# Transfers moved between queues, filler matmuls moved, and one routing stage shifted by a unit in a fused attention and mixture-of-experts kernel

## The reference

```python
# attention: q, k, v of (4, 8, 576, 64)
scores = scale * q @ k.T
scores = np.where(scores >= max(scores) - tau, scores, -1e9)
attn = softmax(scores)                 # over the keys
x = (attn @ v)                         # -> 2304 tokens x 512
# mixture of 8 experts, one expert for each token
logits = (x / |x|) @ (emb / |emb|).T / tau
e = argmax(logits); gate = softmax(logits)[e]
y = gate * (relu(x @ w1[e]) @ w2[e])   # 512 -> 1024 -> 512
# dense block
h = y @ w_in                           # 512 -> 2048
out = (max(h, 0) + alpha * min(h, 0)) @ w_out
```

## Time and profile before

| | us |
|---|---|
| time, median of 3 runs | 1015.94 |
| the three runs | 1015.75, 1015.94, 1016.86 |
| time of the profiled execution | 1015.94 |
| its span (first to last instruction) | 1014.3 |
| PE busy | 1002.7 |
| DVE busy | 528.1 |
| ACT busy | 390.8 |
| POOL busy | 337.4 |

### The profile page before, as it was taken

How to read it: one execution, slowest core, us unless ns; L and a number is a source line. 1 busy time by engine, 2 the same in 40 slices (tenths; PEclk the granted TensorE clock), 3 DMA queues, 4 the chain that set the end, 5 groups by cost and what they waited for, 6 DMA issues and landing times.

```text
span 1014.3 us, 19467 instructions
## 1 busy us (share of the span) xinstructions
PE 1002.7 (99%) x6541; PEld 882.8 (87%) x6542; DVE 528.1 (52%) x1206; ACT 390.8 (39%) x814; POOL 337.4 (33%) x446
## 2 busy tenths in 40 slices
PE   8999999999999999999999999999999999999997
PEld 7988998998988788888888889999899999998996
DVE  6888888888987422222212237544444444444442
ACT  5777777777767232222223223321121211111111
POOL 3333334222131789999954542010010100100101
PEclk9999999999999999999999999999999999999999
DMA  5866776776662555665563335000000000000000
GB/s 133 225 153 167 185 190 172 185 187 174 148 178 52 217 196 203 210 210 192 188 201 128 129 130 155 6 32 32 1 32 32 32 12 19 31 0 0 32 1 31
DMA packets 103744, 116.69 MB, mean 115 GB/s; under 512 B 70380, under 2 KB 70412, under 8 KB 103156
## 3 DMA queue, kind: packets, MB, share of 16 engines
q1 hardware_dynamic: 88404, 87.52, 31.5%
q10 hardware_dynamic: 11120, 13.97, 4.3%
q0 software_dynamic: 4144, 14.20, 3.9%
HBM read 68.53 MB, written 19.12 MB: 86 GB/s over the span
## 4 chain that ended last, share of the span: by engine, by line
PE 95%; POOL 2%; DVE 2%; issue 1%; DMA 0%; ACT 0%; POOLq 0%; SPq 0%; DVEq 0%; ACTq 0%
PE bank L790 82%; PE bank L793 13%; POOL ring L690 1%; DVE neg_max L1563 0%; POOL ring L688 0%; DMA qraw<-in_q 0%; DVE probs L1571 0%; POOLq L89 0%; DVE q_st L1588 0%; POOL x_sorted L731 0%; POOL out L783 0%; DVE k_both L1592 0%; ACT probs L1302 0%; DVE k_st L1592 0%; ACT o_row L1527 0%
## 5 line engine op out<-in xcount | busy, mean ns | idle before, releaser
L790 PE MATMUL bank<-x_hi,ring 128*128 128x384 f32 x768 | 210.5, 337 | 0.0
L790 PE MATMUL bank<-ring,g_hi 128*128 128x512 f32 x576 | 179.1, 392 | 0.0
L1504 ACT ACTIVATE g_hi<-act 128x384 fp32r<-128x384 f32 x96 | 50.4, 525 | 298.9 <-DVE act L1947 296.5
L690 POOL TENSOR_TENSOR ring<-stage,ring 128x2048 fp32r<-128x2048 f32 x32 | 147.2, 4600 | 4.8 <-POOL ring L688 0.2
L790 PEld LDWEIGHTS bank<-x_hi,ring 128*128 128x128 f32 x768 | 140.2, 188 | 3.5
L1944 DVE TENSOR_SCALAR neg<-bank,alpha_col 128x384 f32<-128x384 f32 x96 | 59.2, 617 | 150.8 <-PE bank L790 150.8
L790 PE MATMUL bank<-x_lo,ring 128*128 128x384 f32 x384 | 128.9, 336 | 0.0
L1563 DVE TENSOR_REDUCE neg_max<-bank 128x1 f32<-128x576 f32 x144 | 104.5, 753 | 40.9 <-PE bank L790 39.8
L1302 ACT ACTIVATE probs<-bank,neg_max 128x576 f32<-128x576 f32 x144 | 103.3, 741 | 51.5 <-DVE neg_max L1563 51.4
L790 PEld LDWEIGHTS bank<-ring,g_hi 128*128 128x128 f32 x576 | 106.8, 188 | 18.7 <-DVE g_lo L1895 0.3
L790 PE MATMUL bank<-k_st,q_st 128*128 128x288 f32 (+5 forms) x696 | 114.7, 306 | 0.8 <-DVE probs L1571 0.6
(11 more groups left out here) (204 smaller groups left out, 1406.2 us busy)
## 6 DMA issues: line engine op xcount, KB each, us to landing
stage<-in_moe_w SPq DMA_DIRECT2D x26, 1024.0 KB, 5.3
k_st<-k_both SPq DMA_DIRECT2D x60, 288.0 KB, 4.8
x_row<-x_sorted ACTq DMA_DIRECT2D x23, 296.0 KB, 3.2
stage<-in_moe_w SPq DMA_DIRECT2D x12, 512.0 KB, 5.8
y_sorted<-y_row ACTq DMA_DIRECT2D x21, 256.5 KB, 2.9
q_st<-q_hi SPq DMA_DIRECT2D x30, 160.0 KB, 2.8
q_st<-q_lo SPq DMA_DIRECT2D x30, 160.0 KB, 2.9
qraw<-in_q SPq DMA_DIRECT2D x16, 256.0 KB, 3.1
```

Source lines behind the costliest of these rows:

```text
L690: nc.gpsimd.tensor_tensor(lo, src, hi.bitcast(F32), ALU.subtract).then_inc(piece_lo, 2)
L790: return nc.tensor.matmul(dst, lhsT, rhs, start=start, stop=stop)
L1504: nc.scalar.activation(g_hi[f % 3][:, :], act2[f % 2][:, :], ACT.Copy).then_inc(g_hi_ready, 1)
```

## The change

The changes are these.

- **Start.** The 4 filler matmuls on `vraw` and their semaphore are gone. POOL clears both `vraw` after `qraw` and `kraw`.
- **Unit 0 of pair 0.** The last part of the preparation of pair 1 stood before `turn_last_keys` with 4 fillers behind it. It now stands at the end of the unit, and the 4 fillers are gone.
- **The load of the opening slot** (`x_row`) is issued by SP behind the four loads of `vraw` of pair 15, and no longer by ACT in unit 2 of pair 14.
- **Routing group 2.** Its steps on DVE, its rank on PE and its scatters on POOL each stand one unit later. Two small operations of DVE (`open_gap`, `iota_pos`) move from unit 4 of pair 14 to the end of group 2's steps.
- **After attention.** The zeros of expert 1 and the loads of slots 0 and 1 move from ACT to SP. PE transposes slot 0 (`turn_slot(0)`) behind the whole opening slot, with one filler matmul ahead of it and three behind it.

```diff
+WARM, WARM_SPLIT = 1, 3
...
-STEP_AT = ((0, 1, 2, 3, 4, 5, 6, 8, 8, 9),) * 2 + ((-1, -1, 0, 0, 1, 1, 2, 4, 4, 5),)
-RANK_UNIT = (4, 4, 0)
-SCATTER_AT = ((10, 11, 12, 13),) * 2 + ((6, 6, 7, 7, 8),)
+STEP_AT = ((0, 1, 2, 3, 4, 5, 6, 8, 8, 9),) * 2 + ((0, 0, 1, 1, 2, 2, 3, 5, 5, 6),)
+RANK_UNIT = (4, 4, 1)
+SCATTER_AT = ((10, 11, 12, 13),) * 2 + ((7, 7, 8, 8, 9),)
...
 @block.sync
                     load_v(n + 1, 1 - par)
+                    if n == PAIRS - 2:
+                        sp.wait_ge(scattered_open, 16 * OPEN_TILES)
+                        sp.dma_start(x_row[:, :], x_sorted[0:P, :]).then_inc(open_in, 16)
...
-            for e in (0, *range(2, EXPERTS)):
+            for e in range(EXPERTS):
                 if e == 2:
+                    sp.wait_ge(rows_ready, 1)
+                    rows = [sp.value_load(slot_row[0:1, i:i + 1], ...) for i in range(2)]
+                    for z in range(2):
+                        sp.wait_ge(zeroed[z], 16)
+                    sp.wait_ge(open_turned, 1)
+                    sp.wait_ge(open_squared, 1)
+                    sp.wait_ge(scattered, 16 * (TT - OPEN_TILES))
+                    sp.dma_start(x_row[:, :], x_sorted[ds(rows[0], P), :]).then_inc(xs_in, 16)
+                    sp.wait_ge(table_ready, 1)
+                    sp.dma_start(x_row1[:, :], x_sorted[ds(rows[1], P), :]).then_inc(xs1_in, 16)
                     sp.wait_ge(xs_in, 16)
...
 @block.gpsimd
-            nc.gpsimd.memset(vraw[1][:, MAIN:MAIN + 2, :, :], 0.0).then_inc(fill_ready, 1)
             for t in (*qraw, *kraw):
                 nc.gpsimd.memset(t[:, MAIN, :, :], 0.0)
-            nc.gpsimd.memset(vraw[0][:, MAIN:MAIN + 2, :, :], 0.0).then_inc(const_ready, 1)
+            for t in vraw:
+                last = nc.gpsimd.memset(t[:, MAIN:MAIN + 2, :, :], 0.0)
+            last.then_inc(const_ready, 1)
...
 @block.tensor
-            pe.wait_ge(fill_ready, 1)
-            blank = vraw[1][:, MAIN, :, :].rearrange("p h d -> p (h d)")
-            for _ in range(FILL // 2):
-                mm(bank[:, T_BANK[0], 0:P], blank, blank, True, True)
             pe.wait_ge(const_ready, 3)
...
                     turn_probs(n, j, 0)
-                    if (n, j) == (0, 0):
-                        pe.wait_ge(split_lo, GROUPS_PREP + len(SECOND_BANKS))
-                        prep(1, 1, 0, 2)
-                        busy(FILL // 2, M_BANK)
                     turn_last_keys(n, j)
...
-                    if job and (n, j) != (0, 0):
+                    if job:
...
             open_second(range(0, 4), True)
-            turn_slot(0)
             pe.wait_ge(open_hT_lo, 2)
             open_second(range(4, FC), True, stop=True).then_inc(slots_done, 1)
+            def warm_up(n):
+                for _ in range(n):
+                    mm(bank[:, M_BANK, :], ring[:, 0, 0:P], ring[:, 0, 0:D], True, True)
+            warm_up(WARM)
...
 slot_first(i)
+                if static(i):
+                    turn_slot(0)
+                    warm_up(WARM_SPLIT)
                 pe.wait_ge(piece_lo, e * PIECES + DC)
...
 @block.scalar
-                    if (n, j) == (PAIRS - 2, 2):
-                        act.wait_ge(scattered_open, 16 * OPEN_TILES)
-                        act.dma_start(x_row[:, :], x_sorted[0:P, :]).then_inc(open_in, 16)
...
-                if s == 0:
-                    act.wait_ge(route_const, 9)
-                    act.wait_ge(zero_ready, 1)
-                    row = act.value_load(zero_at[0:1, 1:2], ...)
-                    act.dma_start(x_sorted[ds(row, P), :], zero_row[:, :]).then_inc(zeroed[1], 16)
-                else:
-                    act.wait_ge(rows_ready, 1)
-                    row = act.value_load(slot_row[0:1, 0:1], ...)
...
-            for e in range(2):
-                act.wait_ge(zeroed[e], 16)
-            act.wait_ge(open_squared, 1)
-            act.wait_ge(scattered, 16 * (TT - OPEN_TILES))
-            act.dma_start(x_row[:, :], x_sorted[ds(row, P), :]).then_inc(xs_in, 16)
-            act.wait_ge(table_ready, 1)
-            load_slot(1)
```

More of the change, by code:

```diff
@@ L241, in build @@
         const_ready = sem("const_ready")
-        fill_ready = sem("fill_ready")
         taus_in = sem("taus_in")
@@ L617, in _ @@
             sp.wait_ge(zero_ready, 1)
-            for e in (0, *range(2, EXPERTS)):
+            for e in range(EXPERTS):
                 if e == 2:
+                    sp.wait_ge(rows_ready, 1)
+                    rows = [sp.value_load(slot_row[0:1, i:i + 1], min_val=0, max_val=EXPERTS * CAP + P) for i in range(2)]
+                    for z in range(2):
[6 more added lines that the diff above has]
+                    sp.dma_start(x_row1[:, :], x_sorted[ds(rows[1], P), :]).then_inc(xs1_in, 16)
                     sp.wait_ge(xs_in, 16)
@@ L1046, in open_second @@
                 return last
-            H_BANK, HT_BANK, X_BANK, Y_BANK = (0, 1), (2, 3), 4, 5
-            def turn_slot(i):
-                wait_row(pe, i)
-                if not static(i):
-                    pe.wait_ge(xs_lo, i)
-                row = row_of(i)
-                for c in range(DC):
-                    last = turn(bank[:, X_BANK, c * P:(c + 1) * P], row[:, c * TURNED + EXPERTS:c * TURNED + EXPERTS + P])
-                last.then_inc(xs_turned, 1)
             def turn_params():
@@ L1099, in _, with turn_slot @@
             open_second(range(0, 4), True)
-            turn_slot(0)
             pe.wait_ge(open_hT_lo, 2)
             open_second(range(4, FC), True, stop=True).then_inc(slots_done, 1)
+            def warm_up(n):
+                for _ in range(n):
+                    mm(bank[:, M_BANK, :], ring[:, 0, 0:P], ring[:, 0, 0:D], True, True)
+            warm_up(WARM)
+            H_BANK, HT_BANK, X_BANK, Y_BANK = (0, 1), (2, 3), 4, 5
+            def turn_slot(i):
+                wait_row(pe, i)
+                if not static(i):
+                    pe.wait_ge(xs_lo, i)
+                row = row_of(i)
+                for c in range(DC):
+                    last = turn(bank[:, X_BANK, c * P:(c + 1) * P], row[:, c * TURNED + EXPERTS:c * TURNED + EXPERTS + P])
+                last.then_inc(xs_turned, 1)
             flat = ring[:, :, :].rearrange("p r n -> p (r n)")
@@ L1397, in _ @@
                 nc.scalar.activation(h_row[:, s * D:(s + 1) * D], bank[:, OPEN_H[s], :], ACT.Relu).then_inc(open_relu, 1)
-                if s == 0:
-                    act.wait_ge(route_const, 9)
-                    act.wait_ge(zero_ready, 1)
-                    row = act.value_load(zero_at[0:1, 1:2], min_val=0, max_val=EXPERTS * CAP)
-                    act.dma_start(x_sorted[ds(row, P), :], zero_row[:, :]).then_inc(zeroed[1], 16)
-                else:
-                    act.wait_ge(rows_ready, 1)
-                    row = act.value_load(slot_row[0:1, 0:1], min_val=0, max_val=EXPERTS * CAP + P)
                 act.wait_ge(open_hT, s + 1)
@@ L1686, in route_step @@
                     V.tensor_copy(hot_of(g + 1)[:, 1:EXPERTS, 0], cum_of(g)[:, 1:EXPERTS, nt])
-                    then(V.scalar_tensor_tensor(out=hot_of(g + 1)[:, 0:1, 0], in0=r_open[:, :], scalar=0.0, in1=cum_of(g)[:, 0:1, nt],
-                                                op0=ALU.max, op1=ALU.add))
+                    V.scalar_tensor_tensor(out=hot_of(g + 1)[:, 0:1, 0], in0=r_open[:, :], scalar=0.0, in1=cum_of(g)[:, 0:1, nt],
+                                           op0=ALU.max, op1=ALU.add)
+                    then(V.tensor_scalar(open_gap[:, :], r_open[0:1, :], 0.0, -float(P), ALU.max, ALU.mult))
+                    dve.wait_ge(route, count[0])
+                    then(V.tensor_scalar(iota_pos[:, :], iota_i[:, :], float(P), open_gap[0:1, 0:1], ALU.mult, ALU.add))
             def pair(n, par, half):
@@ L1725, in pair @@
                         constants()
-                    if (n, j) == (PAIRS - 2, UNITS - 1):
-                        dve.wait_ge(route, count[0])
-                        then(V.tensor_scalar(open_gap[:, :], r_open[0:1, :], 0.0, -float(P), ALU.max, ALU.mult))
-                        dve.wait_ge(route, count[0])
-                        then(V.tensor_scalar(iota_pos[:, :], iota_i[:, :], float(P), open_gap[0:1, 0:1], ALU.mult, ALU.add))
                     for g in range(3):
```

## The result

The changed kernel takes 1023.62 us (median of 4 runs, 1022.81 to 1024.05), the kernel before 1016.40 us in the runs beside it (1015.75 to 1016.91). The ratio is 1.0069, 95% interval 1.0055 to 1.0085: 7.2 us slower, where 3.1 us were predicted. The profiled execution of the changed kernel took 1024.61 us; its span is 1022.9 us, 8.6 us more than that of before.

The account below looks back on a forecast made before the run. PE, busy 99% of the span, was taken as the bound. Terms 2.5 (opening slot's load) + 0.6 (start) + 0 + 0 + 0 = +3.1 us on 1015.94 gave 1019.0 us, range 1016.4 to 1021.4.

Parts of the forecast that it names:

- unit 0: Unit 0 of pair 0: removed fillers and moved transposes lie ahead of PE's wait for DVE's probs; 0 us.
- The clock falls: Rival: PE standing about 3 us for x_row may return to 1.2 GHz; price 2 us, 1021.0 us; chance 0.12.
- The load of the opening slot: Pair 14, main term: SP issues x_row later, it lands at 310.4, PE stands 2.6 us; +2.5 us net.
- the scatter's 1.3 us: Pair 14: one more group 2 scatter in the full DMA stretch, 1.3 us more, backlog ending near 310.3.
- The start: Kernel start: later first matmul delays the clock's rise past the q transposes; +0.6 us, bounds 0 and +1.1.
- Group 2: Routing group 2 one unit later: same instructions, DVE has room; 0 us, bounds -0.3 and +0.3.
- After attention: Passage to the slots: slot 0 ends within or close to PE's 0.52 us wait for POOL; 0, bounds 0 and +0.9.
- a sign: Passage to the slots: PE's start of slot 1 would still wait for POOL.
- early landing rival: Pair 14: SP through at 305.6 to 306, rows by 308.8, PE stands 0.5 to 1 us; 1017.2 or 1016.4; chance 0.20.

Follow-up runs that it names:

- b_late_first: Kernel before with routing group 2 one unit later and the opening slot's load by SP ahead of the four vraw loads; 1018.03 us, ratio 1.0015.
- b_load: Kernel before with only the opening slot's load moved to SP, behind the four vraw loads of pair 15; 1018.55 us, ratio 1.0016.
- b_open: Kernel before with the opening slot's load by SP behind the vraw loads and routing group 2 one unit later; 1021.52 us, ratio 1.0051.
- b_unit0: Kernel before with pair 1's last preparation part at the end of unit 0 of pair 0, its 4 fillers gone; 1016.98 us, ratio 1.0016.

## Why the prediction fell short

The forecast was 4.1 us short: 7.2 us were measured and 3.1 predicted. About 1.6 us of this are the clock in unit 0, about 1.6 the clock at the stand, and 0.9 the stand itself (3.4 instead of 2.5).

- **The clock is the step that failed.** "PE idles some 1 us there instead; I expect no fall of the clock from it" was wrong: unit 0 costs 1.6 us alone (0.2 to 3.0), not 0. And the rival *The clock falls* was given 0.12 although its price of 2 us was near the 1.3 to 1.6 measured. The argument against it, that the clock never fell in this trace with a longest stand of 0.73 us, was no evidence about a stand of 3 us, which before never had while there was work. And the same trace has a longer stand, at its end, which the prediction did not look at:

```profile
1007.34 0.39 PE L790 MATMUL bank<-ring,g_lo 128*128 128x512 f32 x1
```

```profile
1012.00:1013.00 1.00, 0.00 (x0) 0.00 (x0) 0.00 (x0) 0.00 (x0) 0.00 (x0) 0.56 0.00 0
```

The first row is PE's last matmul, the second the stretch in which the clock falls, at 1012.1 (from 1011 to 1012 it is still 1.00). That is 4.4 us after the matmul's end (in `b_late_first` 2.1 us after it). So that a stand of some microseconds can bring the clock down could be seen before anything was run. All five profiled executions with a bare stand of 3.3 to 3.7 us for `x_row` show a half clock that begins in the stand or within 0.9 us behind it; the two with 2.3 and 1.4 us do not. Stand and clock should have been one term of 4 to 5 us. As the clock does not fall in every execution, it would still have been a chance and not a certainty.
- **The load of the opening slot** was predicted at +2.5, from a landing at 310.4. The mechanism was right: PE stands for `x_row`, released by the DMA. Its size was too small. The sum held SP's issue at 307.09 and put the scatter's 1.3 us on the landing. The runs show it the other way: SP's issues ahead of the load take 1.1 us longer, and the landing keeps its 3.1 to 3.3 us. `b_load` does land at 310.4 (issue at 307.11, transposes at 310.45, stand 2.26), but without the scatter that the prediction had counted in, so this agreement is luck; with group 2 the stand is 3.4.
- The Trainium skill, "TensorE: Matmul & The Clock Gate", Part 1, says that the slow clock is the default and is returned to when PE idles. The prediction used that page for the start and not for the stand. The stands of 3.4 us agree with it. The same Part 1 tells of a kernel whose short idle times between groups of matmuls made its clock swing; the front of this kernel, with 0.69 and 0.96 us of idle, is nearer to that.
- **The start**: predicted +0.6, measured 0.9 (0.0 to 1.8), and 0.6 as the average of the traces. The size was right, and the reason in the main: with a late first matmul six of seven traces have slow q transposes, with an early one two of ten.
- **Group 2** was priced at 0 ± 0.3 for DVE's steps. No run has it alone; in `b_late_first` 1.5 us were lost and 1.37 of them are the stand, which leaves nothing to speak of for the steps. Its scatters are worth 1.1 us of stand.
- **After attention**: predicted 0, measured 0.7 (-0.2 to 1.6) in and nothing out. Not told from 0. PE no longer waits for POOL at slot 1 in the changed kernel, which the prediction had named as a sign.
- The parts sum to 2.6 + 5.1 + 0.7 = 8.4 us against 7 (5.5 to 8.5) for the whole. That the total is a little less is within the intervals.

The early landing rival fell in every trace with the load behind `vraw`: SP was never through by 306. It had leaned on pair 13, whose twelve issues took 10.2 us; in pair 14 they take 11.4 us in `b_load`, without ACT's load in the way and without the later scatter.

## What to carry to other kernels

Where an edit lets TensorE stand for some microseconds, price the stand and the half clock that can come with it as one term: here 3.4 us of stand cost about 5. Look at the granted clock of each execution and not only at the median: a kernel whose clock falls in half of its executions has two prices. Fillers that look idle because a wait covers them may be what keeps the clock up; before removing them look at how much PE would be idle around them, not at whether they are on the chain. A DMA that is handed to another engine's list takes on everything ahead of it in that list: put it at the place where its data are ready, and the move costs nothing.

## What the runs showed of the hardware

- The clock fell in or just behind stands of 3.3 to 3.7 us in five of five profiled executions (over all executions of `b_open`, in four of five). At the end of the span it fell 4.4 us after PE's last matmul in the kernel before, and 2.1 us after it in `b_late_first`. At the front of the kernel, where PE has two idle times of under 1 us, it fell in six of seven; in one of the six it fell behind the first idle time, of 0.69 us. 14 fillers of 128x128 in a stand kept it at 1.00 in the profiled executions of both kernels that had them.
- While there was work for PE, a half clock lasted 3.4 us in ten of twelve cases, 6.8 us in `b_open` and 10.2 us in `b_unit0`. While it lasts 10 parts of scores take 2.48 us instead of the 1.41 of `b_load`, 1.76 times as long. From the transposes to the scores of eight parts it is 5.46 us in the changed kernel and 6.45 in `b_open`, against 3.86 in `b_load`.
- A load of 128 rows that was issued last in a full stretch landed in 3.1 to 3.3 us in eight traces, against 4.4 to 6.6 us in the eight in which it was issued in the middle of one. The delay was in SP's issues ahead of it, not in its own landing.
